# A recurrent attention kernel with two expert layers: first batch's sign planes, later batches' sums of squares, last batch's weight loads

## The reference

```python
mag = np.sqrt(a_re * a_re + a_im * a_im)
scale = np.minimum(mag, 0.999) / (mag + 1e-06)      # a is scaled by it
S = a[t] * S + k[t] outer v[t];  y[t] = q[t] @ real(S)
```

## Time and profile before

| | us |
|---|---|
| median of 3 runs | 611.38 |
| lowest and highest | 609.99, 617.66 |
| the profiled execution, time | 613.04 |
| its span | 611.3 |
| TensorE busy | 525.0 |
| VectorE busy | 393.0 |
| ScalarE busy | 336.0 |
| GpSimd busy | 138.6 |

### The profile page before, as it was taken

The page is one execution under the profiler, slowest core; times in us unless marked ns, Lnnn a source line. Parts: engine busy times, 40 slices in busy tenths (PEclk is TensorE's granted clock), DMA queues, the critical chain, the costliest instruction groups (busy, mean ns, idle before and its releaser), DMA issues.

```text
span 611.3 us, 11739 instructions
## 1 busy us (share of the span) xinstructions
PE 525.0 (86%) x4572; PEld 394.0 (64%) x4572; DVE 393.0 (64%) x651; ACT 336.0 (55%) x590; POOL 138.6 (23%) x118
## 2 busy tenths in 40 slices
PE   1430569997989798999899998999999999999997
PEld 1210247765667466766787644588888888888886
DVE  5899999999988999796542440599433233233322
ACT  6864624895548942275334312776556555555653
POOL 7000000000000000000000000266655555555553
PEclk9685679996989989999999998999999999999999
DMA  7400656558956488776679999200101001010101
GB/s 274 154 1 0 157 170 144 129 102 217 197 128 156 94 190 272 182 196 130 174 201 259 420 424 423 95 0 2 53 1 53 0 1 51 2 53 1 53 1 51
DMA packets 41607, 79.59 MB, mean 130 GB/s; under 512 B 7376, under 2 KB 29008, under 8 KB 40400
## 3 DMA queue, kind: packets, MB, share of 16 engines
q1 hardware_dynamic: 36944, 65.86, 37.6%
q10 hardware_dynamic: 4608, 12.99, 6.6%
HBM read 55.12 MB, written 4.72 MB: 98 GB/s over the span
## 4 chain that ended last, share of the span: by engine, by line
PE 59%; DVE 20%; ACT 7%; DMA 6%; issue 4%; SPq 2%; ACTq 1%; DVEq 0%
PE ps L1498 10%; PE ps L1494 10%; PE ps L1495 10%; PE ps L1201 8%; DMA stk<-xout 5%; PE ps L1187 3%; PE ps L1468 3%; DVE tt L858 3%; DVE big L864 3%; DVE tt L860 3%; SPq L277 2%; DVE big L832 2%; PE ps L1388 2%; PE ps L1410 2%; DVE xout L954 2%
## 5 line engine op out<-in xcount | busy, mean ns | idle before, releaser
L1166 DVE TENSOR_TENSOR qs<-rs 128x512 f32<-128x512 f32 x96 | 82.6, 860 | 118.9 <-ACT rs L727 118.9
L788 POOL TENSOR_TENSOR hlo<-qs,hhi 128x512 fp32r<-128x512 f32 x96 | 126.3, 1316 | 128.8 <-DVE qs L1166 124.8
L1494 PE MATMUL ps<-hhi,who 128*128 128x512 f32 x285 | 111.0, 389 | 0.0
L1495 PE MATMUL ps<-hhi,wlo 128*128 128x512 f32 x285 | 110.9, 389 | 0.0
L727 ACT ACTIVATE rs<-ps 128x512 f32<-128x512 f32 x96 | 57.4, 597 | 82.3 <-PE ps L1468 82.1
L1187 PE MATMUL ps<-ident 128*32 128x512 bf16 x256 | 74.0, 405 | 31.3 <-DVE xout L954 31.3
L1201 PE MATMUL ps<-stk 112*128 112x224 f32 (+1 forms) x384 | 81.8, 371 | 15.2 <-DMA stk<-xout 15.1
L1201 PEld LDWEIGHTS ps<-stk 112*128 112x128 f32 x384 | 72.6, 206 | 27.2 <-DMA stk<-xout 20.7
L1498 PE MATMUL ps<-hlo,who 128*128 128x512 f32 x285 | 80.5, 390 | 0.1
L780 POOL MEMSET sinz<- 128x768 f32 x1 | 0.7, 738 | 328.1 <-PE ps L1244 328.1
L731 ACT ACTIVATE hhi<-rs 128x512 fp32r<-128x512 f32 x96 | 60.8, 633 | 3.1
(11 more groups left out here) (161 smaller groups left out, 813.8 us busy)
## 6 DMA issues: line engine op xcount, KB each, us to landing
stk<-xout SPq DMA_DIRECT2D x132, 128.0 KB, 3.7
wt<-in_w SPq DMA_DIRECT2D x8, 1536.0 KB, 19.0
big<-in_a_all SPq DMA_DIRECT2D x12, 768.0 KB, 5.3
xq<-in_xq SPq DMA_DIRECT2D x24, 384.0 KB, 4.8
wt<-in_w ACTq DMA_DIRECT2D x12, 768.0 KB, 7.3
vr<-in_v_all SPq DMA_DIRECT2D x24, 192.0 KB, 4.6
out<-ost SPq DMA_DIRECT2D x5, 768.0 KB, 3.5
wins<-in_w_in SPq DMA_DIRECT2D x1, 3072.0 KB, 25.0
```

The costliest lines, as they stand in the source:

```text
L788: pool.tensor_tensor(hlo[:, i % NHS, :], qs[:, i % NQS, :], hhi[:, i % NHS, :].bitcast(F32), ALU.subtract).then_inc(lo_ready, 1)
L1166: dve.tensor_tensor(qs[:, i % NQS, :], rs[:, i % NQS, :], rs[:, i % NQS, :], ALU.mult).then_inc(sq_ready, 1)
L1494: nc.tensor.matmul(accs[k], wh[k], hi, start=(f == 0), stop=False)
L1495: nc.tensor.matmul(accs[k], wl[k], hi, start=False, stop=False)
```

## The change

Three edits.

1. Batch 0: VectorE normalises each tile with three instructions: the first imaginary half, the second imaginary half with its sign turned, and the real plane. ScalarE then makes `N_` of a tile with one negating copy of 768 columns, where it took three copies of 384. It waits for the imaginary part of the tile alone.
2. Batches 2 and 3: the six adds of squares, and the fill-in steps beside them, leave VectorE. GpSimd issues each as a transfer that adds `V_` into `U_` (384 KB, accumulating), once the tile's squares are done. `log_m2` waits for the transfer's landing, on a semaphore for each tile.
3. Period 4: ScalarE's weight loads are issued at the start of a chunk, before its key copies, and not behind its restack; some are one or two chunks earlier.

```diff
+                im = PL[b % 2] + PF + t * PT
+                if b == 0:
+                    act.wait_ge(im_ready, t + 1)
+                    nc.scalar.activation(grid(N_ + t * PT, [1, PT]), grid(im, [1, PT]), ACT.Copy, scale=-1.0).then_inc(signed, 3)
+                    return
...
-                    act.wait_ge(m2_ready, DT * (b - (b > 1)) + t + 1)
+                    if b:
+                        act.wait_ge(m2_added[t], 16 * (b - 1))
+                    else:
+                        act.wait_ge(m2_ready, t + 1)
...
+                    if p == B and c == 1:
+                        act.wait_ge(chain, C_ALL * B)
+                        act.wait_ge(kq_ready, 2 * NC * (B - 1))
+                        load_part(6, 3, 4)
+                        load_part(10, 0, 2)
+                    elif p == B and c == 2:
+                        load_half(8)
+                        load_half(9)
+                    elif p == B and c == 3:
+                        load_half(10)
+                        load_part(5, 0, 2)
+                    elif p == B and c == 4:
+                        load_half(11)
+                        load_part(5, 2, 3)
...
-                    if p == B and c == 1:
-                        act.wait_ge(chain, C_ALL * B)
-                        act.wait_ge(kq_ready, 2 * NC * (B - 1))
-                        load_part(6, 3, 4)
-                    if p == B and 2 <= c < NC:
-                        load_half(NC + c)
-
-                    if p == B and c == 1:
-                        load_part(10, 0, 2)
-                    if p == B and c == 3:
-                        load_part(5, 0, 2)
-                    if p == B and c == 4:
-                        load_part(5, 2, 3)
...
+            for b in range(2, B):
+                for t in range(DT):
+                    pool.wait_ge(squares, DT - 1 + 2 * (DT * (b - 1) + t + 1))
+                    pool.dma_start(grid(U_ + t * PT, [1, PT]), grid(V_ + t * PT, [1, PT]), accum_op=ALU.add).then_inc(m2_added[t], 16)
...
-                if b == 0 and t == DT - 1:
-
-                    for c, done in ((1, im_ready), (0, an_ready)):
-                        dve.scalar_tensor_tensor(out=grid(PL[0] + c * PF + t * PT, [1, PT]), in0=grid(U_ + t * PT, [1, PT]),
-                                                 scalar=KNEE, in1=grid(RAW + c * PF + t * PT, [1, PT]), op0=ALU.subtract,
-                                                 op1=ALU.mult, reverse0=True).then_inc(done, 1)
+                if b == 0:
+
+                    for x, turned, done in ((PF, False, None), (PF + HP, True, im_ready), (0, False, an_ready)):
+                        i, cols = x % PF, HP if x else PT
+                        made = dve.scalar_tensor_tensor(out=grid(PL[0] + x + t * PT, [1, cols]),
+                                                        in0=grid(U_ + i + t * PT, [1, cols]), scalar=KNEE,
+                                                        in1=grid(RAW + x + t * PT, [1, cols]), op0=ALU.subtract,
+                                                        op1=ALU.mult, reverse0=not turned)
+                        if done is not None:
+                            made.then_inc(done, 1)
                     return
...
-                    if 0 < p < B - 1 and 1 <= c < 3:
-                        fill(p)
-                        norm2(p + 1, c - 1)
...
-                    if 0 < p < B - 1 and c == 2:
-                        norm2(p + 1, 2)
```

More of the change, by code:

```diff
@@ L199, in program @@
         kv_done, s_copied, y_done = sem("kv_done"), sem("s_copied"), sem("y_done")
-        m2_summed = sem("m2_summed")
+        m2_summed, m2_added = sem("m2_summed"), [sem(f"m2_added{t}") for t in range(DT)]
         y_copied, x_done, x_copied = sem("y_copied"), sem("x_done"), sem("x_copied")
@@ L469, in sign_planes @@
             def sign_planes(b, t):
-                if b == 0 and t == DT - 1:
[L471 to L474, removed]
+                im = PL[b % 2] + PF + t * PT
[3 more added lines that the diff above has]
+                    return
+                act.wait_ge(an_ready, DT * b + t + 1)
+                if t == 0:
                     act.wait_ge(chain, C_ALL * b)
-                im = PL[b % 2] + PF + t * PT
                 n0, n1 = grid(N_ + t * PT, [1, HP]), grid(N_ + t * PT + HP, [1, HP])
@@ L794, in spot, with norm2 @@
                 return off + j // 2 * 2 * NC + j % 2
[L796 to L801, removed]
+            def norm2(t):
+                dve.wait_ge(squares, min(t + 1, DT - 1))
+                dve.wait_ge(own_squares, t + 1 + (t == DT - 1))
                 u = grid(U_ + t * PT, [1, PT])
@@ L1020, in _ @@
                 first_squares(t)
-                norm2(0, t)
+                norm2(t)
             for t in range(DT):
```

## The result

The changed kernel takes 618.46 us (median of 22 runs, 610.68 to 624.98), the kernel before 611.66 in the same series (22 runs, 605.56 to 620.0). The ratio is 1.0076 [1.0047, 1.0104], which is 2.9 to 6.4 us; by means over all runs it is 617.3 against 612.4, +5.0 ± 1.2 us. The forecast was 608.3 us, a gain of 3.1: sign and size are wrong, and the median lies outside the range of 603.0 to 616.5. The change costs about 1%; that is within 2%, the case to which I gave 0.94, but on the other side.

What follows compares the result with a forecast made beforehand. VectorE sets the early pace, TensorE the stretch from 390 us, with restack transfers on the chain between. Terms -0.9 - 0.9 + 3.6 - 1.0 - 3.9 = -3.1 us, on the median 611.38, give 608.3 us; range 603.0 to 616.5.

Steps and rivals of the forecast that it cites:

- the case to which I gave 0.94: Whole kernel: time stays within 2% (12.2 us) of before, called the same; chance 0.94.
- Head: Batch 0: first product step starts at 22.12 us instead of 23.01, all of it coming through; -0.9 us.
- Six sums off VectorE: Periods 1 and 2: only one add lies ahead of the chain's exit from VectorE, in period 2; -0.9 us.
- The adds as transfers: Periods 1 and 2: transfers hold shared engines 1.2 us an add, delaying awaited restacks; +3.6 us, ends 0 and 7.2.
- count of three adds ahead of a restack: One add ahead of an awaited restack in period 1 and two in period 2, each 1.2 us.
- rival 2: Periods 1 and 2: adds are dear, deciding at 2.2 us each; at 4 us each 616.7 us; chance 0.20.
- the wait at line 417: ScalarE's read of the transferred sum: tightest case leaves 12.4 us, so the wait costs nothing.
- The estimate by the Trainium skill: GpSimd-issued transfer: 2.0 us plus bytes over 436 GB/s, so an add lands in 2.9 us; left the sum unchanged.
- The last period's weights: Period 4: issuing weight loads earlier removes some waits before the experts; -1.0 us, ends -2.6 and +4.5.
- (b): Period 4: weights ahead of restacks need 3.5 and 4.7 us, so restacks of chunks 20 to 22 land about as before.
- Rival 3: Period 4: restacks of chunks 20 to 22 queue behind weights, each 1.5 us late; 613.8 us; chance 0.18.
- The expert stage: Fourth pair's first-layer weights land earlier, removing TensorE's stop (-2.4) and slow matmuls (-1.5); -3.9 us, ends -3.9 and 0.

Runs made afterwards that it cites:

- e1: Kernel before with only batch 0's head change (three normalising instructions, one sign copy a tile): median 607.82 us, ratio 0.9955.
- e5: Kernel before with the six adds of squares left out, done by no engine and no transfer: median 611.02 us, ratio 1.001.
- e15: Kernel before with the six adds as accumulating transfers of only 128x1 (0.5 KB) each: median 610.99 us, ratio 1.0028.
- e12: Kernel before with six plain copies of the same size in place of accumulating transfers: median 614.42 us, ratio 1.0014.
- e2: Kernel before with only the six adds as accumulating GpSimd transfers: median 616.66 us, ratio 1.0007 from its five lowest runs.
- e8: Kernel before with the head change and the earlier weight loads, without the adds as transfers: median 612.04 us, ratio 1.0008.
- e14: Changed kernel with the last period's weight loads moved behind their chunk's state copy, amounts unchanged: median 615.56 us, ratio 1.0062.
- e7: Kernel before with the head change and the new weight amounts, issued behind the chunk's state copy: median 607.25 us, ratio 0.9944.
- e11: e8 with all six restack transfers of the last period's chunks on SyncE's queue: median 612.26 us, ratio 0.9982.
- e13: Kernel before with one GpSimd transfer of 0.5 KB added at its start: median 609.6 us, ratio 1.0008.
- e4: Kernel before with the six adds computed by GpSimd itself, with no transfer: median 614.47 us, ratio 1.0056.

## Why the prediction was wrong

**Head, -0.9: right.** The first product step came at 22.16, forecast 22.12. In e1 the kernel gained at least as much (-2.4 ± 1.0). In after it reaches chunk 1's key and query products and is lost in the restack behind them.

**Six sums off VectorE, -0.9: not shown.** Leaving them out brings 1.1 ± 1.0 by means (e5) and nothing by the ratio; e15, with the same relief, shows +0.1 ± 0.9.

**The adds as transfers, +3.6: mis-sized, and this is the first step that failed.** I said: "I take the plain copy, the only kind that a row prices: 1.2". The price was right for a plain copy (e12: 1.2) and wrong for an accumulation: 2.15. By my own count of three adds ahead of a restack that makes 6.5, inside my ends of 0 and 7.2; measured are 4.4 ± 1.7 to 5.6 ± 1.7 by means (e2 less e15, e2 less e5), and by the ratios 4.2 ± 3.2 (after and e8) and 7.2 ± 3.2 (e14 and e7). The count was off as well: in after chunk 1's restack landed late, as I had it, but in period 2 TensorE didn't wait for chunk 8's. So the traces place some 2 us of the loss, in period 1; where the rest arises stays open. At 2.15 my rival 2, which decides at 2.2, stood at its threshold. What I called "against" it ("even twice the plain copy is only 2.4") was true and should have counted for it: 2.4 lies above 2.2. I had also looked at restacks alone. In period 2 of after ScalarE stood 5.33 us for a raw load, which no step of mine priced; as e1 has a like wait of 3.26 without any add as a transfer, it can't be put down to the adds. That the wait at line 417 would cost nothing held. The estimate by the Trainium skill ("DMA: Bandwidth & Descriptors", Anatomy of one DMA) for a transfer that GpSimd issues, 2.9 us to landing, fails here: the plain copies' median is 4.7 and the accumulations' 6.0.

**The last period's weights, -1.0: wrong in sign, and this is the larger failure.** Edit 3 alone is +1.8 ± 1.0 with the expert stage's gain in it (ratio 1.0027 [0.9991, 1.0064]); against the same kernel with the loads behind the state copy e8 is +6.1 ± 1.8. The step that failed is (b): "At 3.0 us a MB these need 3.5 and 4.7 us, so the restacks of chunks 20 to 22 land about when they do now". It took the loads to run at the full rate from their issue on and to be through when the restack comes. The rate was right (2.6 us a MB), the start was not: issued at 298.69, the loads had 2.4% of the engines until 301, while SyncE's queue, with the restack's first half and another load, had 91.7%; they had 91.9% from 301 to 304, just when ScalarE issued its half of the restack. Rival 3 had the place right; that both share ScalarE's queue, its reason, isn't needed, since e11 has the late restack without it. Its price of 1.5 us each was spread too evenly: chunk 20's restack cost TensorE 2.74 in after and 4.50 in e8, and by the clock the matmuls behind took 6.07 and 5.44 for 3.29; no term of mine had this.

**The expert stage, -3.9: right.** 34.8 for 38.8; stop and cold matmuls both gone. But period 4 gave back what it brought, and I had argued the two apart, though the same bytes are in both: what leaves the full stretch after 335 us goes into the one before it, where restacks are awaited. And the stop isn't in every profile of the old amounts (0.17 us in e2, 0.50 in e13).

**Sum.** With the parts by means, -2.4 (head), +4.5 (edit 2) and +1.8 (edit 3), the sum is +3.9 ± 2.0 against +5.0 ± 1.2 measured. My range missed because I gave its upper end to one dear case at a time. Rivals 2 and 3 don't exclude each other; taken together, at 2.15 an add and 1.5 a restack, my own terms give -3.1 + 2.9 + 5.5 = +5.3. That this meets the measured 5.0 is in part luck: one restack of the last period cost 2.74 and then as much by the clock, where the term has three at 1.5.

## What to carry to other kernels

An add handed to a transfer isn't free: read it as bytes on a shared resource, price it at nearly twice a plain copy, and look for the transfers that an engine awaits beside it. When loads are pulled forward, ask when the engines will be free to start them and which short transfers will be in flight then, in any queue; an issue a few us later in the same list (behind the state copy) took the loss away. Don't put a late transfer down to a change before a kernel without that change has been read at the same place. And when two rivals can both hold, work out their sum before setting the range.

## What the runs showed of the hardware

- An accumulating SBUF-to-SBUF transfer of 384 KB takes 2.15 us of all 16 engines and 864 / 6 = 144 packets (after); the plain one 1.2 us and 80 (e12). One of 0.5 KB has 144 packets as well, and six of them 0.2% of the engines' time (e15).
- A restack transfer of 128 KB that took 3.25 to 3.93 us to land took 5.05 to 5.71 beside such an accumulation, and 8.54 beside weight loads on another queue that held 81.5% of the engines (e11).
- GpSimd's and VectorE's additions get in each other's way while both read two SBUF tiles (e4): 1.95 us for a VectorE instruction of 0.46.
- A wait of 2.74 us on TensorE was followed by 16 matmuls that took 2.78 us longer than after a short wait (6.07 for 3.29). The extra isn't in proportion to the wait: it was 2.15 after 4.50 (e8) and 1.69 after 0.91 (e14), and nothing after 1.16 (e7) or 1.56 (e15).
